# Experts' groups on TensorE in one loop with an empty first pass, with a conditional fourth transpose and a split one-hot build

## The reference, cut to what matters

```python
def _attn_ref(q, k, v, f_logit):            # [4, 8, 768, 48]
    f = 1 / (1 + exp(-f_logit))
    for t in range(S):
        state = f[t] * state + outer(k[t], v[t])
        y[t] = q[t] @ state

def _moe_ref(x, expert_emb, tau, w1, w2):   # x [3072, 384], 8 experts, F = 1024
    logits = normed(x) @ normed(expert_emb).T / tau
    expert_idx = argmax(logits, axis=1)
    for e in range(8):
        mask = expert_idx == e
        out[mask] = gate_w[mask, None] * (relu(x[mask] @ w1[e]) @ w2[e])

def _moe2_ref(x, w_a, w_b, w_out):          # F = 1536
    return ((x @ w_a) * (x @ w_b)) @ w_out
```

## Time and profile before

| | us |
|---|---|
| median of 3 plain runs (830.64 to 831.64) | 831.33 |
| the profiled execution's own time | 830.27 |
| its span, first to last instruction | 829.0 |
| PE busy | 810.1 (98%) |
| DVE busy | 364.4 (44%) |
| ACT busy | 321.6 (39%) |
| POOL busy | 141.1 (17%) |

### The profile page before, as it was taken

The page is one execution under the profiler, slowest core; times in us unless marked ns, Lnnn a source line. Parts: engine busy times, 40 slices in busy tenths (PEclk is TensorE's granted clock), DMA queues, the critical chain, the costliest instruction groups (busy, mean ns, idle before and its releaser), DMA issues.

```text
span 829.0 us, 14425 instructions
## 1 busy us (share of the span) xinstructions
PE 810.1 (98%) x5400; PEld 736.9 (89%) x5401; DVE 364.4 (44%) x597; ACT 321.6 (39%) x608; POOL 141.1 (17%) x206
## 2 busy tenths in 40 slices
PE   5999998989999999999999999999999999999998
PEld 4999987989999999998888888888888888888887
DVE  6788877836453645356532322232232223222221
ACT  5677775435453545355421321231222212212211
POOL 4544440423232322100000100010010001001001
PEclk9999999999999999999999999999999999999999
DMA  9777752556552554320000100010010001000001
GB/s 211 194 207 193 201 176 88 110 192 212 206 174 92 207 199 155 125 77 1 0 1 1 39 1 0 1 39 1 0 39 1 1 1 38 1 1 10 28 1 39
DMA packets 32572, 67.57 MB, mean 82 GB/s; under 512 B 12145, under 2 KB 21390, under 8 KB 31374
## 3 DMA queue, kind: packets, MB, share of 16 engines
q1 hardware_dynamic: 28174, 55.93, 22.0%
q0 software_dynamic: 4352, 11.04, 4.3%
HBM read 57.48 MB, written 9.48 MB: 81 GB/s over the span
## 4 chain that ended last, share of the span: by engine, by line
PE 97%; DVE 1%; issue 1%; DMA 0%; ACT 0%; POOL 0%; DVEq 0%
PE low_banks L1024 18%; PE scores L1024 18%; PE sums L1031 9%; PE high_banks L1031 9%; PE sums L978 8%; PE low_banks L967 6%; PE scores L967 6%; PE high_banks L978 4%; PE scores L812 3%; PE sums L828 3%; PE high_banks L801 2%; PE sums L819 2%; PE low_banks L787 2%; PE low_banks L795 1%; PE high_banks L839 1%; PE sums L901 1%
## 5 line engine op out<-in xcount | busy, mean ns | idle before, releaser
L568 POOL DMA_INDIRECT out<-out_sb,placed x24 | 23.3, 970 | 469.3 <-ACT out_sb L758 463.4
L1024 PE MATMUL low_banks<-x_hi,wab_lo 128*128 128x512 f32 x216 | 84.7, 392 | 0.0
L1024 PE MATMUL scores<-x_hi,wab_lo 128*128 128x512 f32 x216 | 84.7, 392 | 0.0
L1024 PE MATMUL low_banks<-yT_lo,wab_hi 128*128 128x512 f32 x216 | 84.6, 392 | 0.0
L1024 PE MATMUL scores<-yT_lo,wab_hi 128*128 128x512 f32 x216 | 84.6, 392 | 0.0
L1024 PE MATMUL low_banks<-x_hi,wab_hi 128*128 128x512 f32 x216 | 84.0, 389 | 0.0
L1024 PE MATMUL scores<-x_hi,wab_hi 128*128 128x512 f32 x216 | 84.0, 389 | 0.0
L1417 DVE TENSOR_TENSOR h<-low_banks,a_sb 128x512 f32<-128x512 f32 x36 | 25.0, 693 | 132.4 <-ACT a_sb L741 132.4
L1417 DVE TENSOR_TENSOR h<-scores,a_sb 128x512 f32<-128x512 f32 x36 | 25.0, 693 | 130.2 <-ACT a_sb L741 117.9
L741 ACT ACTIVATE a_sb<-low_banks 128x512 f32<-128x512 f32 x36 | 21.6, 599 | 137.8 <-PE low_banks L1024 137.8
L741 ACT ACTIVATE a_sb<-scores 128x512 f32<-128x512 f32 x36 | 21.6, 599 | 134.5 <-PE scores L1024 134.5
(11 more groups left out here) (229 smaller groups left out, 1867.8 us busy)
## 6 DMA issues: line engine op xcount, KB each, us to landing
w_raw<-in_w SPq DMA_DIRECT2D x8, 1536.0 KB
w_raw<-in_w SPq DMA_DIRECT2D x32, 384.0 KB
tok<-in_tok SPq DMA_DIRECT2D x48, 192.0 KB, 3.2
qk_all<-in_chan SPq DMA_DIRECT2D x48, 192.0 KB, 3.3
xd<-xst SPq DMA_DIRECT2D x24, 192.0 KB, 1.9
wab_raw<-in_wab SPq DMA_DIRECT2D x6, 768.0 KB, 6.6
wout_raw<-in_wout SPq DMA_DIRECT2D x1, 1536.0 KB, 6.4
wout_raw<-in_wout SPq DMA_DIRECT2D x1, 768.0 KB, 4.3
```

Of the source, the lines that this page charges most:

```text
L568: pool.indirect_dma_start(out=out, out_offset=bass.IndirectOffsetOnAxis(ap=placed[:, u * B + t, 0:1].bitcast(i32), axis=0), in_=out_sb[:, ...
L1024: last_op = pe.matmul(bank[2 * i + m][:, :], w[:, KM * m + k, cols], moving, start=(k == 0 and w is wab_hi and x is not None), stop=(k == ...
```

## The change

Four things are changed.

PE's experts' code becomes one loop of nine passes. In pass 0 the body is jumped over, and the block at its end waits for `groups_ready`, loads whether group 0 is wide, and does `transpose_x(0)`. In passes 1 to 8 four values are loaded into registers at the head: the group's number `j` (from a new constant table `group_no`), `used`, `chosen` and `following` (whether the next group is wide). The groups above eight come after this loop instead of before it.

`transpose_x` takes `wide`: the fourth tile is transposed only if the group to come is wide; otherwise one product of 32 x 8 raises the semaphore in its place. In the body the branch on `i < FULL - 1` becomes one on `j + 1 < used`.

`in_low` is made by DVE for 15 tiles; for the other nine ACT makes (low - column) squared, nine instructions of 128 columns, and then relu(1 - that) over all 1,152 columns. PE waits for that one before its last nine products of L942.

POOL makes the new constant table, and waits, before the gather of a fourth tile, for the previous gather into it; `tile_wide` has an unused first column.

```diff
@@ constants, POOL
+            pool.memset(group_no[:, 0:1], 0)
+            pool.iota(group_no[:, 1:], pattern=[[1, FULL]], base=0, channel_multiplier=0)
@@ gather_x, POOL
                     pool.wait_ge(x1T_done, j * TB - TB + t + 1)
+                    if t == TB - 1:
+                        pool.wait_ge(xin_loaded[t], j * 16)
@@ ACT, after the norm
+        act.wait_ge(low_known, 1)
+        for i in range(BY_DVE, TILES):
+            act.activation(off[:, i - BY_DVE, :], column[:, :], ACT.Square, bias=r["low"][:, i:i + 1], scale=-1.0).then_inc(rest_ready, 1)
+        act.wait_ge(rest_ready, TILES - BY_DVE)
+        act.activation(in_low[:, BY_DVE:, :], off[:, :, :], ACT.Relu, bias=1.0, scale=-1.0).then_inc(rest_ready, 1)
         for i in range(PAIRS):
             w1_high(0, i)
@@ PE
         for i in range(TILES):
-            pe.wait_ge(low_ready, i + 1)
+            if i < BY_DVE:
+                pe.wait_ge(low_ready, i + 1)
+            else:
+                pe.wait_ge(rest_ready, TILES - BY_DVE + 1)
...
-        def transpose_x(j, fill=0):
-            for t in range(TB):
+        def transpose_x(j, wide, fill=0):
+            def tile(t):
                 pe.wait_ge(xin_loaded[t], j * 16 + 16)
                 for k in range(KM):
                     last_op = pe.transpose(bank[t][:, P * k:P * k + P], xin[:, t, P * k:P * k + P], ident[:, :])
                 last_op.then_inc(x1T_done, 1)
+
+            for t in range(TB - 1):
+                tile(t)
                 keep_warm(fill)
+            if wide is None:
+                tile(TB - 1)
+            else:
+                with pe.If(wide > 0):
+                    tile(TB - 1)
+                with pe.If(wide < 1):
+                    pe.matmul(bank[TB - 1][0:32, 0:E], every[:, 0:32], every[:, 0:E], start=True, stop=True).then_inc(x1T_done, 1)
...
-        def group(j, n, i):
+        def group(j, n, used, following):
             up(j, n)
             pe.wait_ge(y_copied, j * KM + 1)
             down(j, 0, n, True)
-            with pe.If(i < FULL - 1):
-                transpose_x(j + 1)
+            with pe.If(j + 1 < used):
+                transpose_x(j + 1, following)
             for m in range(1, KM):
                 down(j, m, n, False)
 
-        transpose_x(0, fill=3)
-        pe.wait_ge(groups_ready, 1)
+        with pe.Fori(0, FULL + 1) as i:
+            with pe.If(i > 0):
+                j = pe.value_load(group_no[0:1, bass.ds(i, 1)], min_val=0, max_val=FULL - 1)
+                used = pe.value_load(tiles_used[0:1, 0:1], min_val=FULL, max_val=NT)
+                chosen = pe.value_load(tile_wide[0:1, bass.ds(i, 1)], min_val=0, max_val=1)
+                following = pe.value_load(tile_wide[0:1, bass.ds(i + 1, 1)], min_val=0, max_val=1)
+                pe.wait_ge(x1l, j * TB + TB)
+                with pe.If(chosen < 1):
+                    group(j, 3 * P, used, following)
+                with pe.If(chosen > 0):
+                    group(j, TW, used, following)
+            with pe.If(i < 1):
+                pe.wait_ge(groups_ready, 1)
+                following = pe.value_load(tile_wide[0:1, 1:2], min_val=0, max_val=1)
+                transpose_x(0, following, fill=3)
         more = pe.value_load(tiles_used[0:1, 2:3], min_val=0, max_val=NT - FULL)
+        used = pe.value_load(tiles_used[0:1, 0:1], min_val=FULL, max_val=NT)
         with pe.If(more > 0):
-            with pe.Fori(0, NT - FULL) as j:
-                with pe.If(j < more):
+            with pe.Fori(FULL, NT) as j:
+                with pe.If(j < used):
                     pe.wait_ge(x1l, j * TB + TB)
-                    group(j, TW, 0)
-        with pe.Fori(0, FULL) as i:
-            j = i + more
-            chosen = pe.value_load(tile_wide[0:1, bass.ds(j, 1)], min_val=0, max_val=1)
-            pe.wait_ge(x1l, j * TB + TB)
-            with pe.If(chosen < 1):
-                group(j, 3 * P, i)
-            with pe.If(chosen > 0):
-                group(j, TW, i)
+                    group(j, TW, used, None)
@@ DVE
-        link(dve.tensor_copy(r["low"][:, :], place_low[:, :]))
+        dve.tensor_copy(r["low"][:, :], place_low[:, :]).then_inc(low_known, 1)
+        dve.wait_ge(low_known, 1)
...
-        for i in range(TILES):
+        for i in range(BY_DVE):
             dve.tensor_scalar(in_low[:, i, :], column[:, :], r["low"][:, i:i + 1], None, ALU.is_equal).then_inc(low_ready, 1)
...
-        dve.tensor_scalar(tile_wide[:, :], r["left"][:, :], 3.0 * P, None, ALU.is_gt).then_inc(groups_ready, 1)
+        dve.tensor_scalar(tile_wide[:, 1:], r["left"][:, :], 3.0 * P, None, ALU.is_gt).then_inc(groups_ready, 1)
```

More of the change, by code:

```diff
@@ L54, in attention_moe_ffn @@
     EARLY = TILES - B
+    BY_DVE = 15
     assert 2 + C <= FULL
@@ L82, in attention_moe_ffn @@
     tile_no = sb("tile_no", [P, NT])
+    group_no = sb("group_no", [P, 1 + FULL], i32)
     tile_start = sb("tile_start", [P, NT])
@@ L94, in attention_moe_ffn @@
     tile_begin = sb("tile_begin", [P, NT], i32)
-    tile_wide = sb("tile_wide", [P, NT], i32)
+    tile_wide = sb("tile_wide", [P, 1 + NT], i32)
     tiles_used = sb("tiles_used", [P, 3], i32)
@@ L186, in attention_moe_ffn @@
         r[name] = sb("r_" + name, shape)
+    off = sb("off", [P, TILES - BY_DVE, P], f16)
     r["pre"] = sb("r_pre", [P, 1 + E * TILES], f16)
@@ L265, in attention_moe_ffn @@
         sem, ("norm_ready", "ex_ready", "diff_ready", "prefix_ready", "rank_done"))
+    low_known, rest_ready = map(sem, ("low_known", "rest_ready"))
     low_ready, inverted, token_ready, tokenT_done, table_ready, table_stored = map(
```

## The result

| | before | after |
|---|---|---|
| median (runs) | 830.99 us (4) | 840.93 us (4: 840.0 to 842.81) |
| span of the profiled execution | 829.0 | 838.4 |
| PE busy | 810.1 | 810.7 |

The account below looks back on a forecast made before the run. PE, busy 98% of the span, was taken to bound the kernel. Terms 4.1 - 1.8 + 7.6 - 0.1 - 1.1 = +8.7 us gave 840.0 us against the median 831.33; range 831.0 to 846.0, likeliest case 836 to 845.

Parts of the forecast that it names:

- How far the sequencer is ahead: Between groups of the experts' loop: PE's full queue gives a lead of 3.26 us after narrow groups, 3.66 after wide.
- 18.8 products: End of group 1: the sequencer's lead of 3.26 us at 0.173 us a product; 18.7 after wide group 3.
- Rival (c): Head of each pass: the loads hide if the lead is above 4.4 us; faster, 828.2 us; chance 0.13.
- The four loads: Head of each pass: sequencer needs 4.3 us against 3.26; group 0 to 1 -1.8 us, six others +7.6.
- Pass 0: Before group 0: jump to unread code and loads no longer hidden; first product at 159.3 for 155.18, +4.1 us.
- The second wait for code: Block behind pass 0's jump, some 75 instructions, may run into absent code: between 0 and 4.48, taken as 2.2 us.
- rival (b): Group 0's products: the clock falls after little PE work from 150.4 to 159.3; 3.4 us more, 843.4; chance 0.12.
- Fourth tile: In-loop transposes for groups 1, 2, 5, 6: 4 x (0.33 - 0.05), -1.1 us; bounds -1.3 and -0.8.
- One-hot rows: Routing before token: nine fewer rows on DVE, nine on ACT; -0.1 us, between -1.2 and +1.3.
- Rival (e): Behind group 0: the empty pass does not cure L1005's first branch; +3.2 less 1.4, 842; counted within the forecast's range.

## Why the prediction was right

The forecast was 840.0 (831 to 846) with 0.81 on slower; 840.93 came.

**How far the sequencer is ahead.** Right. The 18.8 products at two speeds were the whole case: with three added loads the holes came out within 0.1 us of the 3.26's sums, with one there were none, and the lead is 3.29 us in the kernel after. Rival (c), that the loads hide, fell.

**The four loads.** Forecast 4.3 us between narrow bodies; it is 209.5 to 213.8 in the trace after. Holes forecast at 1.1, with the weights 1.4; they are 1.15 and 1.4 (narrow to narrow), 1.73 for 1.65 (before wide), 0.99 for 0.86 and 0.73 for 0.7 (behind wide). The 0.86 is a slip of the sum: the branch more of 0.26 makes it 0.96 by the prediction's own terms. The six made +8.0 for +7.6, the seventh -1.6 for -1.8. Where they come from is shown from three sides: added to the kernel before, taken out of the kernel after (with two branches), and, alone and with all branches kept, moved within it.

**Pass 0.** The sum, +4.1, was somewhat large; the start came 3.24 later, with the split in it. The first part was right (a branch of 4.23 us for 4.48, at 146.8 for 148.1). The second wait for code, taken as 2.2 us, did not show, though in the kernel with the third tile's branch it is there, 2.59 us. In its place something came that the forecast had only as rival (b), and there for a later time. PE stood still from 149.3 to 151.87, to 150.22 for the gather of the tokens (the row `DMA xin`), then for the branch and the load behind it. The granted clock was half for 152.0 to 154.5 (stretch, length, busy us of PE, PEld, DVE, ACT, POOL, clock, DMA):

```profile
152.00:154.50 2.50, 2.50 (x13) 2.50 (x14) 0.56 (x1) 0.49 (x1) 0.00 (x0) 0.50 0.22 2
```

So the first two tiles and their fillers took 3.56 us (0.90, 1.28, 0.64, 0.74) instead of 2.0. The head's four loads then set the start, as forecast. That 2.2 was put down for a wait that did not come and 1.6 for a clock that was not in the sum is why the term is near; this part was luck.

**Fourth tile.** Wrong in size: -0.2 for -1.1. The step that failed is 4 x (0.33 - 0.05). The small product has its place in the chain for 0.11, not 0.05, and the down products behind it take 4.36 instead of 4.19. Without it they take 4.16 to 4.19 (in the three kernels without it above, which keep two branches on `wide` one tile earlier). Whether it is the product's type (16 bits between fp32 ones), its weights of 32 columns, or the place of the branches just ahead of it, was not tried apart.

**One-hot rows.** Forecast -0.1 on `token` (the prediction's own times, 144.4 for 144.62, give -0.2); it comes 0.59 earlier behind `r["low"]` (138.09 to 143.75, for 138.37 to 144.62). The rows of ACT's squares are as estimated (2.72 us for nine); the last nine products were the term that was too large: 0.40 us in all. The start of group 0 gained 0.72 us from it in one trace and 0.17 in another; alone it moves the time by less than can be told.

Part by part the spans stand so: start +4.0 forecast and +3.24 measured, holes +5.8 and +6.4, tiles -1.1 and -0.2; the sum +8.7 and +9.4. The error at the start and that of the tiles nearly cancel, so the sum is closer than its parts, and that too is luck.

The empty pass in itself: it does what it is made for, the hole of the first branch is gone from behind group 0. But the 4.2 us come back ahead of the first transposes, where PE's fillers end at 149.3, and with the clock they cost 3.35 of start. The kernel without it is no slower. Rival (e), that the pass does not cure that branch, fell.

## What to carry to other kernels

Register loads and branches on TensorE's sequencer were free here only as long as their sum between two bodies stayed under the lead of its queue (3.26 to 3.66 us): measure that lead (the time from the sequencer's first instruction behind a body to the end of the body's products), and put loads where products are queued ahead, not at a loop's head. A branch or loop end that takes microseconds once and a fifth of one later was a wait for code here: look at when the block of code comes, and at what is skipped and how far the program runs straight ahead of it, before adding a pass to warm it. A hole has a second price, as the clock may fall behind it.

## What the runs showed of the hardware that was not expected

Code that is never executed made the kernel 2.2 us faster, by moving what lies behind it. A branch that waited for code ended 1.36 to 1.40 us after the block's packet in six places, and the loop's code, once there, was not fetched again in eight passes.

A hole of the same length is at times followed by half clock. Behind the 2.90 us of the kernel before, and the 2.96 with the split rows, the clock stayed whole; behind 2.70 with three added loads it did not. With one load added, the stretches around a hole of 2.84 read (stretch, length, busy us of PE, PEld, DVE, ACT, POOL, clock, DMA):

```profile
182.00:185.00 3.00, 0.21 (x2) 0.00 (x0) 0.00 (x0) 0.53 (x1) 0.00 (x0) 1.00 0.02 5
185.00:190.00 5.00, 4.95 (x19) 4.96 (x20) 1.49 (x2) 1.26 (x2) 0.00 (x0) 0.66 0.16 29
```

It cost 1.5 to 1.6 us a time in four traces and 2.8 in the one with the moved loads. One kernel's times go with the mean granted clock: of the ten runs with the moved loads, six at 0.996 took 829.7 to 831.1, the four at 0.990 to 0.994 took 832.5 to 835.9. What decides between them was not found.
